# A fused linear attention and two MLPs: rotating two of three chunks first, with the scatter on one queue and the casts ahead of the decay steps

## The reference

```python
mag = sqrt(a_re**2 + a_im**2); scale = minimum(mag, 0.999) / (mag + 1e-6)
for t in range(S):                       # 768 tokens, 4 batches, 8 heads of 48
    S_re, S_im = ar*S_re - ai*S_im + k v^T, ar*S_im + ai*S_re
    y[t] = q S_re
x  = y                                   # 3072 tokens x 384
g  = h * clip(h + 3, 0, 6) / 6           # h = x @ w_in (384 x 2048)
x2 = g @ w_out                           # 2048 x 384
out = ((x2 @ w1) * (x2 @ w2)) @ w3 @ w_out2   # 1024 wide
```

## Time and profile before

| | |
|---|---|
| median of 3 runs | 1017.98 us (1017.22 to 1024.38) |
| the profiled execution | 1022.37 us |
| its span in the trace | 1020.6 us |
| TensorE busy | 910.4 us, 89% |
| VectorE busy | 470.5 us, 46% |
| ScalarE busy | 430.5 us, 42% |
| GpSimd busy | 256.6 us, 25% |
| mean granted TensorE clock | 0.946 |

### The profile page before, as it was taken

How to read it: one execution, slowest core, us unless ns; L and a number is a source line. 1 busy time by engine, 2 the same in 40 slices (tenths; PEclk the granted TensorE clock), 3 DMA queues, 4 the chain that set the end, 5 groups by cost and what they waited for, 6 DMA issues and landing times.

```text
span 1020.6 us, 14665 instructions
## 1 busy us (share of the span) xinstructions
PE 910.4 (89%) x5721; PEld 834.9 (82%) x5721; DVE 470.5 (46%) x610; ACT 430.5 (42%) x650; POOL 256.6 (25%) x200
## 2 busy tenths in 40 slices
PE   6944469889989989989989989989999999999996
PEld 3534468879889889889889889989888888888886
DVE  6445549849658648648748733233212121212110
ACT  4543535555655655555555532353212122212121
POOL 1011336222222222222222222343222222222221
PEclk9977769989989999999999999999999999999999
DMA  9584132353343343343344141510101010101000
GB/s 347 201 230 128 46 63 78 85 119 88 108 87 95 100 91 98 93 90 99 107 89 110 48 84 50 188 68 11 44 1 62 1 62 1 62 1 62 1 32 33
DMA packets 73688, 85.85 MB, mean 84 GB/s; under 512 B 6928, under 2 KB 59792, under 8 KB 73616
## 3 DMA queue, kind: packets, MB, share of 16 engines
q1 hardware_dynamic: 73216, 84.07, 29.7%
q10 hardware_dynamic: 400, 0.80, 0.5%
HBM read 45.22 MB, written 11.01 MB: 55 GB/s over the span
## 4 chain that ended last, share of the span: by engine, by line
issue 39%; PE 38%; POOL 14%; DVE 3%; ACT 2%; DMA 2%; SPq 1%; ACTq 0%; POOLq 0%; DVEq 0%
POOL gL L1328 13%; PE hb L937 10%; PE acc L959 7%; PE bQ L937 5%; PE bR L937 5%; PE bP L959 2%; PE hb L796 2%; PE acc L816 2%; PE acc L890 2%; DMA F<-QKs 1%; PE hb L890 1%; DVE QKc L1198 1%; DMA wo_sb<-in_moe_w_out_dram 1%; PE bQ L846 0%; PE bR L846 0%
## 5 line engine op out<-in xcount | busy, mean ns | idle before, releaser
L1328 POOL TENSOR_TENSOR gL<-g_sb,gH 128x384 fp32r<-128x384 f32 x128 | 157.1, 1227 | 428.2 <-ACT gH L1036 425.9
L796 PE MATMUL hb<-xHL,winH 128*128 128x384 f32 x768 | 168.6, 356 | 10.7 <-DMA xHL<-yHL 9.1
L816 PE MATMUL acc<-gH,woutH 128*128 128x384 f32 x384 | 134.0, 349 | 32.5 <-POOL gL L1328 23.6
L1237 DVE SCALAR_TENSOR_TENSOR g_sb<-t_sb,hb 128x384 f32<-128x384 f32 x128 | 70.4, 550 | 189.6 <-ACT t_sb L1046 105.8
L796 PEld LDWEIGHTS hb<-xHL,winH 128*128 128x128 f32 x768 | 140.2, 199 | 13.3 <-DMA xHL<-yHL 9.5
L1046 ACT ACTIVATE t_sb<-hb,cst 128x384 f32<-128x384 f32 x128 | 74.4, 581 | 154.1 <-PE hb L796 153.4
L816 PE MATMUL acc<-gH,woutL 128*128 128x384 f32 x384 | 133.3, 347 | 0.0
L816 PE MATMUL acc<-gL,woutH 128*128 128x384 f32 x384 | 132.8, 346 | 0.0
L1341 POOL TENSOR_TENSOR pL<-p_sb,pH 128x512 fp32r<-128x512 f32 x48 | 67.0, 1396 | 231.9 <-ACT pH L1098 231.9
L816 PEld LDWEIGHTS acc<-gH,woutH 128*128 128x128 f32 x384 | 75.0, 195 | 37.6 <-issue 29.3
L1036 ACT CAST gH<-g_sb 128x384 fp32r<-128x384 f32 x128 | 65.3, 510 | 79.4 <-DVE g_sb L1237 79.2
(11 more groups left out here) (148 smaller groups left out, 1715.9 us busy)
## 6 DMA issues: line engine op xcount, KB each, us to landing
QKs<-in_qk_x_dram SPq DMA_DIRECT2D x16, 576.0 KB, 4.2
xHL<-yHL SPq DMA_DIRECT2D x48, 144.0 KB, 2.7
F<-QKc SPq DMA_DIRECT2D x16, 292.5 KB, 4.7
AR<-in_a_re_x_dram SPq DMA_DIRECT2D x8, 576.0 KB, 3.9
AI<-in_a_im_x_dram SPq DMA_DIRECT2D x8, 576.0 KB, 4.8
v_sb<-in_v_dram SPq DMA_DIRECT2D x24, 192.0 KB, 2.5
x_dram<-x_sb SPq DMA_DIRECT2D x24, 192.0 KB, 4.1
out_dram<-o_sb SPq DMA_DIRECT2D x6, 768.0 KB, 4.3
```

The lines of the kernel that those rows point to most:

```text
L796: mm = pe.matmul(o, w[:, kk * DF1 + ft * P:kk * DF1 + (ft + 1) * P], xv(u)[:, 2 * kk + part, :], start=(i == 0), stop=(i == 8))
L816: mm = pe.matmul(acc[m][:, 0:UNIT], w[:, ft * DM + m * P:ft * DM + (m + 1) * P], gg[:, (n % 3) * UNIT:(n % 3 + 1) * UNIT], start=(ft == 0 ...
L1237: dve.scalar_tensor_tensor(out=g_sb[:, :], in0=t_sb[:, :], scalar=6.0, in1=hb[n % 2][:, 0:UNIT], op0=ALU.min, op1=ALU.mult).then_inc(s["hs ...
L1328: pool.tensor_tensor(gL[:, (n % 3) * UNIT:(n % 3 + 1) * UNIT], g_sb[:, :], gH[:, (n % 3) * UNIT:(n % 3 + 1) * UNIT].bitcast(F32), ALU.subt ...
```

## The change

It touches only the order and the pieces of the work, not the mathematics. In the order of the diff:

- Decays and the products by cosine and sine are done for the unit's first two chunks (`pair`) and then for the third (`last`), each with semaphores of its own. q and k are loaded together, two chunks and then one (`load_pair`, `load_last`).
- The chain's steps are packed into t = 0 to 14: the cosine and sine by ScalarE come at t = 11 instead of 13, the products for the pair at t = 12 instead of 14 and 15, and those for the third chunk at 13 and 14.
- ScalarE makes gH ahead of the slot's chain step, where before it made it behind (`high_g`).
- SyncE issues both halves of every `scatter_pair` at t = 12 and `load_a` of the next unit at t = 13, where before it issued `load_a` at t = 12 and the scatter at 14 and 15. In unit 0 the sine half was ScalarE's, and is SyncE's now.
- Unit 1's chain begins in slot 9 of u = -1, behind the three chunks of unit 0, where before it was spread over slots 0 to 8. In u = 0 the chain of unit 2 falls one slot later than before, t = sl - 3.
- Copies of w3's rows and the pieces of the first MLP's weights are sorted anew, and the second MLP's weights are loaded two slots sooner and split in six half pieces.

```diff
-        ORDER_W = (0, 4, 1, 5, 2, 6, 3, 7)
-        SPLIT_H = {(-1, 0): (0,), (-1, 8): (4,), (-1, 9): (1,), (0, 1): (5,), (0, 3): (2,), (0, 5): (6,), (0, 7): (3,), (0, 9): (7,)}
-        SPLIT_L = {(-1, 1): (0,), (-1, 8): (4,), (-1, 9): (1,), (0, 1): (5,), (0, 3): (2,), (0, 5): (6,), (0, 7): (3,), (0, 9): (7,)}
+        ORDER_W = (0, 1, 4, 2, 5, 3, 6, 7)
+        SPLIT_W = {(-2, 15): (0,), (-1, 3): (1,), (-1, 8): (4,), (0, 0): (2,), (0, 2): (5,), (0, 4): (3,), (0, 6): (6,), (0, 8): (7,)}
...
             if u == -1:
-                return ([(1, 0)] if sl == 0 else []) + ([(1, sl + 1)] if sl < 9 else [])
+                return {9: [(1, 0), (1, 1)], 10: [(1, 2), (1, 3)], 11: [(1, 4), (1, 5)], 12: [(1, 6)], 13: [(1, 7), (1, 8)],
+                        14: [(1, 9)], 15: [(1, 10)]}.get(sl, [])
             if u == 0:
-                return {0: [(1, 10), (1, 11)], 1: [(1, 12), (1, 13)], 2: [(1, 14), (1, 15)],
-                        3: [(2, 0), (2, 1)], 15: [(2, 13), (2, 14), (2, 15)]}.get(sl, [(2, sl - 2)])
-            return [(u + 2, sl)] if u + 2 < NU else []
+                return {0: [(1, 11)], 1: [(1, 12)], 2: [(1, 13), (1, 14)],
+                        15: [(2, 12), (2, 13), (2, 14)]}.get(sl, [(2, sl - 3)])
+            if u == 1 and sl < 2:
+                return [(3, 0), (3, 1)] if sl else []
+            return [(u + 2, sl)] if u + 2 < NU and sl < 15 else []
...
-        W3_COPY = {(-2, 9): (0, 1), (-2, 10): (2,), (-2, 11): (3, 4), (-1, 0): (5,), (-1, 1): (6,), (-1, 2): (7,)}
+        W3_COPY = {(-2, 8): (0, 1), (-2, 9): (2,), (-2, 10): (3, 4), (-2, 14): (5, 6), (-2, 15): (7,)}
...
                 if p > 0:
-                    sp.wait_ge(s["k_decayed"], p)
+                    sp.wait_ge(s["last_decayed"], 2 * p)
...
+            def load_pair(p):
                 if p == 0:
                     sp.wait_ge(s["pads_cleared"], 1)
                 else:
                     sp.wait_ge(s["f_pair_dma"], 16 * FD * p)
+                    sp.wait_ge(s["kT_psum"], 2 * (carried(CPU * p - 2) + 1))
+                sp.dma_start(qk(QKs)[:, 0:2 * KT, 0:2 * P], qk_src(p)[:, 0:2 * KT, :]).then_inc(s["pair_dma"], 16)
+
+            def load_last(p):
+                if p > 0:
                     sp.wait_ge(s["f_last_dma"], 16 * FD * p)
-                sp.dma_start(qk(QKs)[:, :, 0:P], qk_src(p, 0)).then_inc(s["q_dma"], 16)
-
-            def load_k(p):
-                if p > 0:
                     sp.wait_ge(s["kT_psum"], 2 * carried(CPU * p))
-                sp.dma_start(qk(QKs)[:, :, P:2 * P], qk_src(p, 1)).then_inc(s["k_dma"], 16)
+                sp.dma_start(qk(QKs)[:, 2 * KT:3 * KT, 0:2 * P], qk_src(p)[:, 2 * KT:3 * KT, :]).then_inc(s["last_dma"], 16)
...
                     for p, t in steps(u, sl):
-                        if t == 12 and p + 1 < NU:
+                        if t == 12:
+                            scatter_pair(sp, p, 0)
+                            scatter_pair(sp, p, 1)
+                        if t == 13 and p + 1 < NU:
                             load_a(p + 1)
-                        if t == 14:
-                            scatter_pair(sp, p, 0)
-                        if t == 15 and p > 0:
-                            scatter_pair(sp, p, 1)
                     if sl == 3 and u >= 1:
...
-                if t == 15 and p == 0:
-                    scatter_pair(act, 0, 1)
...
+                        high_g(n)
                         if sl == 1 and u > 0:
                             evac_x2_act(act, u - 1)
-                    if n is not None:
                         for p, t in steps(u, sl):
                             pre(p, t)
-                        high_g(n)
                     if (g := chunk(u, sl, "TK")) is not None and not last_of_batch(g):
                         act.wait_ge(s["kT_psum"], 2 * carried(g) + 1)
...
-                    if u == NU - 1 and sl in (4, 6, 8):
-                        i = sl // 2 - 2
+                    if u == NU - 1 and 3 <= sl < 9:
+                        i, part2 = divmod(sl - 3, 2)
                         act.wait_ge(s[f"mlp2_w_dma{i}"], 16)
-                        act.copy(w2parts[i][0][:, :], w2parts[i][2][:, :]).then_inc(s["mlp2_w_high"], 1)
+                        act.copy(half(w2parts[i][0], part2), half(w2parts[i][2], part2)).then_inc(s["mlp2_w_high"], 1)
...
+                    dve.wait_ge(s["pair_dma"], 16 * (p + 1))
+                    for i, grow in enumerate((AI, AR)):
+                        dve.tensor_tensor(pair(part(QKs, i)), pair(part(QKs, i)), pair(tokens(grow)), ALU.mult).then_inc(s["pair_decayed"], 1)
...
-                if t == 14:
-                    dve.wait_ge(s["q_decayed"], p + 1)
-                    dve.wait_ge(s["k_decayed"], p + 1)
+                if t == 12:
+                    dve.wait_ge(s["pair_decayed"], 2 * (p + 1))
                     dve.wait_ge(s["cos_turns"], p + 1)
                     for i in range(2):
-                        dve.tensor_tensor(part(QKc, i), part(QKs, i), tokens(W3), ALU.mult).then_inc(s["cos_rotated"], 1)
-                if t == 15:
+                        dve.tensor_tensor(pair(part(QKc, i)), pair(part(QKs, i)), pair(tokens(W3)), ALU.mult).then_inc(s["pair_cos"], 1)
                     dve.wait_ge(s["sin_turns"], p + 1)
                     for i in range(2):
-                        dve.tensor_tensor(part(QKs, i), part(QKs, i), tokens(W2), ALU.mult).then_inc(s["sin_rotated"], 1)
+                        dve.tensor_tensor(pair(part(QKs, i)), pair(part(QKs, i)), pair(tokens(W2)), ALU.mult).then_inc(s["pair_sin"], 1)
+                if t == 13:
+                    dve.wait_ge(s["last_dma"], 16 * (p + 1))
+                    for i, grow in enumerate((AI, AR)):
+                        dve.tensor_tensor(last(part(QKs, i)), last(part(QKs, i)), last(tokens(grow)), ALU.mult).then_inc(s["last_decayed"], 1)
+                if t == 14:
+                    dve.wait_ge(s["last_decayed"], 2 * (p + 1))
+                    for i in range(2):
+                        dve.tensor_tensor(last(part(QKc, i)), last(part(QKs, i)), last(tokens(W3)), ALU.mult).then_inc(s["last_cos"], 1)
+                    for i in range(2):
+                        dve.tensor_tensor(last(part(QKs, i)), last(part(QKs, i)), last(tokens(W2)), ALU.mult).then_inc(s["last_sin"], 1)
+
+            def pair(v_):
+
+                return v_[:, :, 0:2, :]
+
```

95 lines of the change are left out of this document (45 added, 50 removed).

## The result

The changed kernel takes 1103.93 us (median of 4 runs, 1101.96 to 1107.16), the kernel before in the same comparison 1017.6 us (1016.12 to 1024.38). The ratio is 1.0837, with a 95% interval of 1.0782 to 1.0893: slower. The direction was forecast, the size was not: 1065 us was predicted, with a range up to 1090. The profiled execution took 1104.54 us, its span 1102.7 us, with a mean granted clock of 0.919 (0.946 before).

A forecast was written before the change was run, and what follows sets the result against it. The decay chain, not TensorE's own work, was taken to set the pace at each new unit. Terms 6 + 6 + 36 + 2 - 3 = +47 us, from the median of 1018, gave 1065 us, range 1018 to 1090.

The forecast's parts named there:

- the term behind y_low: From the last chunk's y_low to the next unit's first scores: 24 us instead of 25.1, 1 us given back per unit.
- the first turn: From first scores of u = 0 to u = 1: products and late load fall in slot 15, +6 us, 0 to 10.
- the start: Up to first scores of u = 0: unit 1's chain begins later, scores at 149 instead of 142.98, +6 us, 3 to 9.
- the stretch ahead of y_low: First scores to the last chunk's y_low: more work on VectorE and ScalarE makes y_low 10.2 us later per unit.
- the last turn: First scores of u = 5 to u = 6, no chain behind it, scores need only F: +2 us, -5 to +5.
- the last weights: Second MLP's weights in halves hold VectorE and ScalarE half as long in a slot: -3 us, -5 to 0.
- Rival 1: Faster: the chain isn't the pace and half the waits for gL and F go, 25 us, 993 us; chance 10%.
- rival 2: The delays fit into the waits, y_low some 4 us late: +5 to +10 us, 1025 us, no change; chance 13%.
- Rival 3: Slower still: load queues behind the scatter, TensorE at its lower clock more often, 1092 us; chance 12%.
- the end of the bracket without a queue: AI's landing behind y_low if the load doesn't queue behind the scatter: 18.0 us.
- the late end of the bracket: AI's landing if the load starts only behind the scatter's last bytes: 22.1 us at most behind y_low.
- gH ahead of the chain's step: On ScalarE: takes away waits for gL, given nothing; some 2 us per turn if the F wait went.

The follow-up runs named there:

- e1: Changed kernel with AR and AI issued ahead of the pair's scatter on SyncE: 1081.68 us, ratio 1.0608.
- e2: Changed kernel with steps 0 and 1 of the next chain moved from slot 0 to slot 2, steps 2 to 4 in slots 3 and 4: 1079.86 us.
- e4: Kernel before with AR and AI of the next chain issued behind both halves of the scatter: 1086.74 us, ratio 1.0661.
- e9: Changed kernel with gH copied behind the chain's step again: 1079.84 us, ratio 1.0573.
- e7: Kernel before with gH copied ahead of the chain's step on ScalarE in each slot: 1043.15 us, ratio 1.0223.
- e3: Changed kernel with y_low of the last chunk ahead of the pair's four products on VectorE: 1091.56 us, ratio 1.0708.
- e12: Changed kernel with load ahead of scatter, y_low ahead of the pair's products, unit 1's chain spread from slot 0, gH behind the chain's step: 1029.27 us.
- e13: The kernel of e12 with unit 2's chain one slot earlier in u = 0: 1026.08 us, ratio 1.0045.
- e11: Kernel before with the last weights in halves, loaded at slot 13, and the change's tables for the first stretch: 1009.68 us, ratio 0.9871.
- e6: Kernel before with the second MLP's weights in six half pieces, loaded at slot 13: 1012.39 us, ratio 0.9936.

## Why the prediction was wrong in size

The trace is 82.1 us longer where the sum said 47. Of the 35 us between them, 20 are the term behind y_low in four turns, 8 the first turn, 7.5 the start, 3 the stretch ahead of y_low, 2 the last turn, and the last weights take 5.5 off.

**Right.** The loop that sets the pace, its order on SyncE and ScalarE, and the places to look: squares released by AI's DMA with 10.8 us of idle time, the first scores of the four turns no longer released by F, y_low behind four products. Up to 123 us the start went as laid out, 3 us late: third chunk's y_low at 90.9 (said 88), chain from 91.5 (88.6), g_sb behind it at 123.2. Rival 1 (the chain isn't the pace) fell with e1, e2 and e4, rival 2 with the distances of 89 to 91 us. Rival 3 lay nearest: the load lands late, and the clock is lower, 9.4 us of busy time in four turns.

**The step that failed most, behind y_low: the term -1, measured +3.9.** Two numbers of it failed. The landing of AI was put 18.0 us behind y_low, the end of the bracket without a queue; it lay 19.9 to 21.0 behind, since the load takes 7.2 us from issue to landing in the median here, where it took 4.8 in the earlier trace rows. The page's rows of the changed kernel:

```profile
AR<-in_a_re_x_dram SPq DMA_DIRECT2D x8, 576.0 KB, 6.3
AI<-in_a_im_x_dram SPq DMA_DIRECT2D x8, 576.0 KB, 7.2
```

And from the squares to the scores I had counted two squares and "some 3 us", 5.4; it is 7.9 (509.33 to 517.19). I had taken the scores to wait for Kc. In fact TensorE stops one step sooner, at the output sums that need `x_sb`, and must still run nine of those products at the lower clock, 3.0 us, before it comes to the scores. Against 18.0 and 5.4 that is +2.3 and +2.5 a turn; and the 25.1 from which I subtracted was one turn, the mean of the four is 24.3. The Trainium skill, "DMA: Bandwidth & Descriptors" (Queues, rings and completion order), was cited for the late end of the bracket, 22 us, by which the load starts behind the scatter. The landing at 20 lies between the two ends. It doesn't show the rule either, since in e1, where AI is issued ahead of the scatter and behind `store_x`, it lands 6.3 us after its issue in the median and not 4.8. Which end a bracket is taken from should have gone by the rows of the new neighbours: a load with a scatter beside it is not the load of the earlier trace rows.

**Ahead of y_low: +10.2 predicted, +10.9 measured, one part by its rows and one by luck.** From the end of g_sb of slot 10 to y_low the four turns take 19.0 us in the mean, where I had laid out 18.8. The other part, how much later that g_sb ends, is 5.1 us (42.5 behind the first scores instead of 37.4), where I had taken 4.9 out of 8.4 as what doesn't fall into slack. No row stood behind that share, and it came out by luck: with gH behind the step (e9) the 5.1 us are 2.7, so nearly half of them come from a term that I had put at nothing.

**The other step that failed: gH ahead of the chain's step, put at nothing, measured 24 us.** I had written that it takes away waits for gL "inside a loop that waits for F later anyway, so I give it nothing", and even saw 2 us a turn to be won. e9 gives 3.5 us ahead of y_low in each of four turns, 5.7 in the first turn and 5.0 in the last; e7 gives 23 us for it in the kernel before. The prediction asked what a wait of TensorE is worth and not what stands behind gH on ScalarE. The loop that waits for F *is* that chain, and gH first puts each of its steps behind a wait for VectorE. The products ahead of y_low cost 3.0 us a turn (e3), and about 4 are left in e12 (54.7 against 50.6 before), which were not taken apart.

**The start: +6 predicted, +13.5 measured.** Behind the 3 us by which the chain began late, two terms were short. The pair's products by the cosine took 5.03 us at 132.72 where I had set 1.8, and the load lands 7.1 us after its issue:

```profile
132.72 5.03 DVE L1194 TENSOR_TENSOR QKc<-QKs,W 128x768 f32<-128x768 f32 x2
```

The scatter began at 137.8 instead of 131.6, and AI landed at 153.7 instead of 146. The row for the price of the products stood in the earlier trace rows (5.84 us beside GpSimd's work), and I cited it and took the short one.

**The first turn: +6 predicted, +14.2 measured.** gH first is 5.7 of it (e9). The table of u = 0, with the chain a slot later and three steps in slot 15, is 4.2 (e13, before what is given back). Against e11, which has the change's weight tables and a turn of 70.3 us, the loss is 21 us, and 11 of it stay open.

**The last turn and the last weights.** +2 was +4.0, and gH first is all of it: e9's last turn is 74.3 us, the kernel before's 75.3. The halves gave -8.5 instead of -3: I had priced them by the longest wait of TensorE in the earlier trace rows, and left out the rest. e6 gives -7.4 in that stretch by the halves and the earlier load alone.

**The range.** Its upper end was the sum of the upper ends of my terms plus nothing for the terms that I had set to zero. One of these measured 24 us.

## What to carry to other kernels

When an instruction is moved ahead of another on an in-order engine, ask what the engine would have done in the wait that now comes first: a step that fills a gap is free there, and behind the wait it lengthens the loop in each round (by 3.5 us a turn here). A load for the next round is ordered by who stands behind its first reader, not by when its data are used: here a reader at the head of ScalarE's queue turned its own wait of 10.8 us for a DMA into one of 10.6 us on TensorE. And a part that looks like nothing in a bundle should be run by itself: of this change two parts paid (1.3%), and the rest hid them.
